# Two fused gated layers behind an attention, one core: when ScalarE and GpSimd round the weights, and in which order ScalarE works in the first step

## The reference, cut to what matters

```python
qn = q / (norm(q, axis=1) + 1e-6);  kn = k / (norm(k, axis=1) + 1e-6)     # norms over the 6016 rows
a  = softmax(kn.T @ qn / tau)                                             # 256 x 256
x  = v @ a                                                                # 6016 x 256
h  = x @ w_in1                                                            # 6016 x 2048
g1 = (a0 + a1*h + a2*h**2 + a3*h**3) / (1 + |b0|*|h| + |b1|*h**2 + 1e-6)
x  = g1 @ w_out1                                                          # 6016 x 256
h  = x @ w_in2
g2 = h * clip(h + 3, 0, 6) / 6
out = g2 @ w_out2
```

## Time and profile before

| | |
|---|---|
| median of the runs | 1113.65 us |
| profiled execution, its own time | 1112.29 us |
| its span, from first to last instruction | 1110.5 us |
| busy: TensorE, VectorE, ScalarE, GpSimd | 1096.3, 894.9, 867.5, 777.5 us |
| mean granted TensorE clock | 0.998 |
| step 0 on TensorE | from 52.2 to about 101 us |

### The profile page before, as it was taken

One profiled execution on the slowest core, in us unless ns is written; L12 is line 12 of the kernel. 1 busy time (PEld: TensorE's weight loads), 2 busy tenths in 40 slices (PEclk: granted clock), 3 DMA queues, 4 the chain that ended last, 5 costly groups with the idle time before them and its releaser, 6 DMA issues.

```text
span 1110.5 us, 16094 instructions
## 1 busy us (share of the span) xinstructions
PE 1096.3 (99%) x5012; PEld 920.3 (83%) x5012; DVE 894.9 (81%) x1288; ACT 867.5 (78%) x1461; POOL 777.5 (70%) x624
## 2 busy tenths in 40 slices
PE   9998999999999999999999999999999999999998
PEld 8887788888888888888888888888888888888887
DVE  6799999987887887887888888888888788787632
ACT  6899888877877877887887877877877787787643
POOL 0489788777777776677777777677777777666643
PEclk9999999999999999999999999999999999999999
DMA  9931010010110110010020011011011010010010
GB/s 347 316 118 20 1 20 1 15 20 1 20 20 1 20 20 1 15 23 0 0 33 5 0 19 19 0 19 19 1 19 20 1 20 1 1 20 1 1 19 19
DMA packets 105464, 33.81 MB, mean 30 GB/s; under 512 B 92982, under 2 KB 98742, under 8 KB 105398
## 3 DMA queue, kind: packets, MB, share of 16 engines
q1 hardware_dynamic: 104832, 32.52, 11.7%
q10 hardware_dynamic: 566, 0.52, 0.1%
HBM read 26.87 MB, written 6.16 MB: 30 GB/s over the span
## 4 chain that ended last, share of the span: by engine, by line
PE 93%; DVE 4%; ACT 1%; issue 1%; DMA 0%; POOL 0%; SPq 0%; DVEq 0%; ACTq 0%
PE H L476 15%; PE H L477 15%; PE H L478 15%; PE YP L476 7%; PE YP L477 7%; PE YP L478 7%; PE OP L477 7%; PE OP L476 7%; PE OP L478 7%; PE OP L507 3%; DVE H L1006 1%; DVE T L999 1%; DVE g_hi L1014 1%; PE OP L676 1%; PE OP L680 1%
## 5 line engine op out<-in xcount | busy, mean ns | idle before, releaser
L423 POOL TENSOR_TENSOR SQ<-SQ,AB 128x512 f32<-128x512 f32 x175 | 231.1, 1320 | 246.5 <-ACT SQ L806 246.2
L437 POOL TENSOR_TENSOR g_lo<-R,g_hi 128x512 fp32r<-128x512 f32 (+1 forms) x191 | 243.8, 1276 | 28.8 <-ACT g_hi L838 28.8
L429 POOL TENSOR_TENSOR g_lo<-SQ,Y 128x512 fp32r<-128x512 f32 (+1 forms) x192 | 244.7, 1274 | 7.9 <-DVE SQ L1042 7.9
L804 ACT ACTIVATE AB<-H,absb 128x512 f32<-128x512 f32 x175 | 120.7, 690 | 141.7 <-PE H L478 141.7
L999 DVE TENSOR_TENSOR T<-T,H 128x512 f32<-128x512 f32 (+1 forms) x192 | 129.2, 673 | 77.9 <-ACT T L812 77.0
L1014 DVE SCALAR_TENSOR_TENSOR g_hi<-H,coef,Y 128x512 fp32r<-128x512 f32 (+1 forms) x192 | 141.5, 737 | 57.0 <-ACT Y L825 56.3
L1048 DVE SCALAR_TENSOR_TENSOR R<-R,H 128x512 f32<-128x512 f32 (+1 forms) x192 | 128.2, 667 | 35.4 <-ACT R L831 35.2
L831 ACT ACTIVATE R<-H 128x512 f32<-128x512 f32 (+1 forms) x192 | 113.5, 591 | 52.3 <-PE H L478 51.6
L476 PE MATMUL H<-vT_hi,wf_hi 128*128 128x512 f32 (+1 forms) x384 | 149.5, 389 | 4.8 <-DVE SQ L1042 2.6
L476 PE MATMUL YP<-g_hi,wd_hi 128*128 128x512 f32 (+1 forms) x384 | 149.4, 389 | 4.0 <-POOL g_lo L429 4.0
L1006 DVE SCALAR_TENSOR_TENSOR H<-T,coef,H 128x512 f32<-128x512 f32 (+1 forms) x192 | 143.0, 745 | 6.8
(11 more groups left out here) (123 smaller groups left out, 2084.2 us busy)
## 6 DMA issues: line engine op xcount, KB each, us to landing
qk<-in_q SPq DMA_DIRECT2D x22, 256.0 KB, 5.6
qk<-in_k SPq DMA_DIRECT2D x22, 256.0 KB, 6.6
v_blocks<-in_v SPq DMA_DIRECT2D x88, 64.0 KB, 2.3
out<-o_tok SPq DMA_DIRECT2D x80, 64.0 KB, 1.8
wd_raw<-in_moe_w_out SPq DMA_DIRECT2D x8, 512.0 KB, 8.3
wu_raw<-in_moe_w_in SPq DMA_DIRECT2D x4, 512.0 KB, 7.5
w_raw_a<-in_moe_w_in SPq DMA_DIRECT2D x2, 1024.0 KB, 11.0
qk<-in_q SPq DMA_DIRECT2D x3, 128.0 KB, 2.9
```

Source lines behind the costliest of these rows:

```text
L423: nc.gpsimd.tensor_tensor(SQ[:, j % 4, 0:w], SQ[:, j % 4, 0:w], AB[:, j % 2, 0:w], ALU.add)\
L429: nc.gpsimd.tensor_tensor(g1_lo[:, j % 4, 0:w], SQ[:, j % 4, 0:w], Y[:, j % 2, 0:w], ALU.mult)\
L437: nc.gpsimd.tensor_tensor(g2_lo[:, j % 4, 0:w], R[:, j % 2, 0:w], g2_hi[:, j % 4, 0:w].bitcast(fp32), ALU.subtract).then_inc(g2_lo_done, 1)
```

## The change

Four edits, none of which adds or removes an instruction.

1. Setup: quarter 2 of w_out1 is rounded behind the norms' root, no longer ahead of it, and unit 1 of w_in2 behind the two Exps.
2. Step 0: ScalarE's order in a slot is root, Abs, square of the root, Square, T, where it was root, square of the root, Abs, Square, T. For that `q_terms` is cut in `q_term` (the Abs) and `q_square`. Other steps keep their order.
3. v's halves are rounded (ScalarE) and split (GpSimd) in slots 7 and 11 of each step, no longer in 6 and 10. VectorE's transposes stay in 6 and 10.
4. Units 6 and 7 of w_in2 move from slots 7 and 9 to 9 and 13, and the eight units of w_out2 from 11, 12, 14, 15, 18, 27, 29, 30 to 19, 20, 22, 24, 26, 28, 30, 32.

In the diff, the first part is the lists, the second stands in the step of GpSimd and in that of ScalarE, the third is ScalarE's setup, the fourth ScalarE's step.

```diff
-    WU2_AT = 3, 5, 7, 9
-    WD2_AT = 11, 12, 14, 15, 18, 27, 29, 30
+    V_SPLIT_AT = 7, 11
+    WU2_AT = 3, 5, 9, 13
+    WD2_AT = 19, 20, 22, 24, 26, 28, 30, 32
...
-                    if j in V_AT and exists(t) and exists(t + 1):
-                        vT_split(t + 1, V_AT.index(j), 1 - par)
+                    if j in V_SPLIT_AT and exists(t) and exists(t + 1):
+                        vT_split(t + 1, V_SPLIT_AT.index(j), 1 - par)
...
-            for part in range(3):
-                wd1_round(part)
+            wd1_round(0)
+            wd1_round(1)
             act.wait_ge(norms_summed, 1)
             nc.scalar.activation(roots, sums, ACT.Sqrt).then_inc(roots_taken, 1)
             nc.scalar.activation(small[:, 41:42], ones[:, 0:1], ACT.Exp)
+            wd1_round(2)
             wd1_round(3)
             wu2_round(0)
-            wu2_round(1)
...
                 nc.scalar.activation(wf_hi[:, :, columns(n)], folded, ACT.Copy).then_inc(fold_hi, 1)
+            wu2_round(1)
...
-                    if x := stage(t, j - LAG_DIVIDE):
+                    x = stage(t, j - LAG_DIVIDE)
+                    if x and isinstance(t, int) and t == 0:
                         root(*x)
+                        q_term(t, j)
                         root_squared(*x)
-                    if exists(t):
-                        q_terms(t, j)
+                        q_square(t, j)
                         p_start(t, j)
+                    else:
+                        if x:
+                            root(*x)
+                            root_squared(*x)
+                        if exists(t):
+                            q_term(t, j)
+                            q_square(t, j)
+                            p_start(t, j)
```

More of the change, by code:

```diff
@@ L791, in _, with q_term @@
             act.wait_ge(root_b1_exact, 1)
-            def q_terms(t, j):
+            def q_term(t, j):
                 w = width(t)
@@ L804, in q_terms, with q_square @@
                 nc.scalar.activation(term, h, ACT.Abs, scale=absb[:, 0:1])
+            def q_square(t, j):
+                w = width(t)
                 wait_chunk(act, g1_lo_done, back(t, j, 4))
-                nc.scalar.activation(SQ[:, j % 4, 0:w], h, ACT.Square, scale=root_b1).then_inc(q_done, 1)
+                nc.scalar.activation(SQ[:, j % 4, 0:w], h1(t, j), ACT.Square, scale=root_b1).then_inc(q_done, 1)
             def p_start(t, j):
```

## The result

The changed kernel takes 1114.6 us (median of 19 runs, 1114.22 to 1115.86), the kernel before 1112.89 in the same session (19 runs, 1111.41 to 1113.79): a ratio of 1.0016, 95% interval 1.001 to 1.0023, so 1.1 to 2.6 us slower, 1.8 by the ratio. The profiled execution took 1114.4 us, with a span of 1112.6.

The account below looks back on a forecast made before the run. It took TensorE, 99% busy, as the bound, so only delays before its stream becomes gapless count. Terms 0 + 0.0 + 0 + 0.75 made +0.75 us, 1114.4 by the median; range 1111.7 to 1116.5.

Parts of the forecast that it names:

- signs of being wrong: No wait behind slot 21, or slot 16 coming over 0.7 us earlier or later than before.
- Part 1: Setup: moving the quarter behind the norms' root and the unit behind the Exps changes nothing, 0.
- Part 2: Step 0, Abs between root and square: odd slots' quotient waits, 0.7 us lost (0.3 in slot 5, 0.2 each in 9, 13).
- Part 3: Step 0, rounding moved out: 1.3 us gained (0.35 in slot 8, 0.2 each in 4 and 12, 0.55 at slot 15's root).
- the 0.55 at the end: Slot 15's root, freed from waiting for GpSimd's g_lo behind a unit's lower half, starts 0.55 us earlier.
- Net of step 0: Step 0 in all: 0.7 - 0.15 - 0.55 = 0.0 us, between -1.6 and +1.5.
- Slots 16 to 19: Moved unit gains nothing, as a slow-clock stretch losing 1.7 us of work covers it: 0, bounds -1.7 and 0.
- Part 4: Step 1, eight w_out2 units: GpSimd delays VectorE's product and the bank's release, 0.75 us lost, bounds 0 and 3.
- The price of the first slot: Step 1: the first slot where GpSimd's added work meets VectorE's product delays the bank's release 1.1 to 1.25 us.
- The second: Slot 23's wait: VectorE's next product waits out GpSimd's sum of slot 22, some 0.7 us, or just precedes it; 0.5 taken.
- The runs of three: Slots 22 to 24 and 26 to 28, each with a unit or half: 1.74 us against slack, 0.1 for both.
- v's halves in the other steps: Rounding and splitting v one slot later in all other steps costs nothing.

Follow-up runs that it names:

- setup_only: Kernel before with only the setup edit (quarter of w_out1 behind the norms' root, unit 1 of w_in2 behind the Exps); 1112.70 us, ratio 1.0002 to the kernel before.
- order_only: Kernel before with only ScalarE's new order in step 0, lists and setup as before; 1113.92 us, ratio 1.0009 to the kernel before.
- order_back: Changed kernel with ScalarE's old order in step 0, lists and setup still changed; 1113.58 us, ratio 1.0005 to the kernel before.
- act_part: Changed kernel with ScalarE rounding only 8 columns of each w_out2 unit, GpSimd still subtracting whole units; 1114.57 us (1 run).
- after_filled: Changed kernel with small unread matmuls, 5 and 8, in TensorE's two idle stretches of slots 17 and 18; 1113.37 us, ratio 1.0007 to the kernel before.

## Why the prediction was right

It forecast 0.75 us slower, 1114.4; measured were 1.8 by the ratio, 1114.6. The way and the mechanisms hold; the sum came to less than half of what was measured. That the medians agree within 0.2 is luck: the kernel before was at 1112.89 in 19 runs, not at the 1113.65 of three, and this error of 0.76 made up for most of the 1.0 that the sum was short. One of its own signs of being wrong did come true: slot 16 is 0.86 late, over the 0.7 that it allowed. Slot 17, on which the rest hangs, is 0.36 late.

- **Part 1: 0, right** (setup_only, and the distance root to Exp in the changed kernel is 4.01 too).
- **Part 2: the mechanism right, the term mis-sized.** I had 0.3, 0.2 and 0.2 lost in slots 5, 9 and 13, by the timeline of slot 9 alone, in which the quotient would be just 0.1 late. Measured were 0.53, 0.58 and 0.33. Once the even slot is faster, VectorE arrives earlier in the odd one and waits longer, and T's wait of 0.12 comes on top. With what slots 4, 8 and 12 gained, the lateness in slot 14 is 0.64, against 0.7 - 0.15 = 0.55 in the sum.
- **Part 3: the gains are there, their causes and the end were wrong.** 1.3 of gains given; slots 4, 8 and 12 gained 0.11, 0.29 and 0.16, slots 15 and 16 0.14 and 0.33: 1.04 on VectorE. But order_only has the gains of the even slots with the old lists, and the lists alone (order_back) give 0.22 of their 0.57: part 2 is enough for them. And "the 0.55 at the end is safe" is the step that failed: from slot 14 to slot 17 TensorE's starts make good 0.28 (0.64 to 0.36), where the lists alone make good 0.71 and the new order alone loses 0.21 (0.66 to 0.87). The root of slot 15 starts 0.2 behind its sum, not within 0.1.
- **Net of step 0:** given 0.0, measured +0.36, inside -1.6 to +1.5; the missing part is that end. The order alone gives +0.87 and the lists alone -0.86, so 0.35 is what the two don't add up to.
- **Slots 16 to 19: right for the difference.** The lower clock costs about 1.0 of TensorE's start of slot 20, not 1.7; the changed kernel has it in all 19 executions, the kernel before in about three of four.
- **Part 4: right in place and cause, too small.** Given 0.15 in slot 22 and 0.5 in slot 23, measured 0.23 and 0.86. The price of the first slot was right, 1.16 by the distances above against 1.1 to 1.25. The second was mis-sized: I took 0.7 for the wait and two in three for its chance, but a `product` that starts 0.03 us behind GpSimd's sum waits for all of it, 1.81 - 0.69 = 1.12, less what slack was left. Nor was it chance: in order_back, act_part and after_filled, which have the unit in slot 20 too, `product` starts 0.04 to 0.06 us behind that sum and takes 1.79 to 1.81. The runs of three cost 0.09 in slot 24, and 0.19 in slots 32 and 33, given 0.1.
- **v's halves in the other steps: 0, right;** the lateness is 1.79 in slot 34 and in the last slot.

## What to carry to other kernels

An instruction put into another's wait brings its own wait along: before moving it look at whose result it needs in each slot, not on the average. When two edits go in together, run each alone: here one of them already had the gain that was put down to the other. Work moved to an engine with idle time is free only while it doesn't push that engine's instructions onto those of a neighbour that then wait for their end, as VectorE's did here; read the duration of the neighbour's instruction in slots with such work and without. And when the chain through TensorE is as long as VectorE's, a gain in one slot is waited for in the next, so take the sum over a pair of slots and not that of the slots.

## What the hardware showed that I had not expected

- A VectorE instruction with both inputs in SBUF doesn't run slower beside a GpSimd subtraction or product that is under way, it waits for its end: started 0.03 us behind a GpSimd sum of 1.29 us it took 1.81 instead of 0.69, and in 362 cases out of 362 it ended 0.54 to 0.56 us behind GpSimd's end. With up to 0.16 us of GpSimd's instruction left it took 0.69 to 0.70. It holds the other way too: the GpSimd sum that was started meanwhile, at 128.56, shows 1.74 instead of 1.29. Whether a memset under way would hold it up, no run shows.
- Ten of the eleven profiles without extra matmuls show a stretch at a granted clock of 1.2 GHz, of 3.4 us and in two of them 6.8, which starts between 108.7 and 118.1 us; that of order_only shows none. In four of them it starts behind TensorE's second long idle stretch (2.3 us), in six already behind the first (1.7 to 2.1 us) or in its last 0.4 us. 13 small matmuls put into the two idle stretches, 1.28 and 1.95 us in all, went with a mean granted clock of 0.999 or 1.000 in all 33 executions of the three kernels that had them, and with a start of slot 20 that was 1.0 to 1.2 us earlier.
